# Second mixture: POOL no longer waits for its gather, and PE waits for the gathered rows itself

## The reference, cut to what matters

```
def _moe2_ref(x, w_skip, w_gate, w1, w2):          # x: 1536 x 512, 8 experts
    do_compute = (x @ w_skip) > 0
    out = x.copy()
    xc = x[do_compute]
    logits = xc @ w_gate
    e_idx = np.argmax(logits, axis=1)
    ... gate_w = softmax(logits)[e_idx]
    for e in range(8):
        mask = e_idx == e
        h = np.maximum(xc[mask] @ w1[e], 0.0)      # w1[e]: 512 x 1024
        y[mask] = gate_w[mask, None] * (h @ w2[e]) # w2[e]: 1024 x 512
    out[do_compute] = xc + y
```

## Time and profile before

| what | value |
|---|---|
| median of 3 runs | 729.18 us (725.63 to 731.9) |
| the profiled execution, its own time | 726.76 us |
| its span in the profile | 724.9 us |
| busy in the span | PE 90%, DVE 52%, ACT 40%, POOL 28% |
| second mixture | from 517.8 us to the end of the span |

### The profile page before, as it was taken

One profiled execution on the slowest core, in us unless ns is written; L12 is line 12 of the kernel. 1 busy time (PEld: TensorE's weight loads), 2 busy tenths in 40 slices (PEclk: granted clock), 3 DMA queues, 4 the chain that ended last, 5 costly groups with the idle time before them and its releaser, 6 DMA issues.

```text
span 724.9 us, 13743 instructions
## 1 busy us (share of the span) xinstructions
PE 653.6 (90%) x4192; PEld 577.0 (80%) x4192; DVE 375.6 (52%) x731; ACT 292.9 (40%) x503; POOL 205.8 (28%) x227
## 2 busy tenths in 40 slices
PE   5786884699999999999999999999699998999992
PEld 4675773389999999999999999976478876777771
DVE  2684697736364546345463645402574576636621
ACT  2362673024343444343343534405065474644620
POOL 0537580130241506051332415030022232221321
PEclk9898997599999999999999999999799999999997
DMA  9999996026272735537192827357355678557221
GB/s 192 204 223 237 267 291 230 20 80 206 75 215 68 185 132 126 201 80 247 50 258 68 219 73 187 129 97 217 96 198 179 178 255 268 152 146 261 44 43 16
DMA packets 94867, 116.16 MB, mean 160 GB/s; under 512 B 55940, under 2 KB 56068, under 8 KB 94800
## 3 DMA queue, kind: packets, MB, share of 16 engines
q1 hardware_dynamic: 77264, 90.83, 41.5%
q0 software_dynamic: 10464, 23.81, 15.7%
q10 hardware_dynamic: 7072, 0.71, 0.8%
HBM read 100.01 MB, written 20.18 MB: 166 GB/s over the span
## 4 chain that ended last, share of the span: by engine, by line
PE 57%; DMA 20%; SPq 8%; issue 7%; DVE 4%; POOLq 1%; POOL 1%; ACT 1%; DVEq 0%; ACTq 0%
PE bank L797 20%; PE bank L791 20%; DMA out<-y_sb,ix_put 10%; DMA xg<-x_moe,ix_take 8%; SPq L502 6%; PE bank L648 3%; PE bank L780 2%; PE bank L769 2%; SPq L517 2%; PE bank L720 2%; PE bank L698 1%; PE bank L681 1%; PE bank L710 1%; PE bank L898 1%; PE bank L670 1%
## 5 line engine op out<-in xcount | busy, mean ns | idle before, releaser
L1462 DVE TENSOR_TENSOR w_lo<-stage,w_hi x120 | 141.5, 1221 | 19.3 <-ACT w_hi L1022 17.4
L1022 ACT CAST w_hi<-stage x120 | 119.6, 1047 | 9.5 <-PE bank L898 9.4
L797 PE MATMUL bank<-unit_hi,w_hi 128*128 128x416 f32 x256 | 92.6, 362 | 0.0
L791 PE MATMUL bank<-tok_hi,w_hi 128*128 128x416 f32 x256 | 90.4, 353 | 0.0
L797 PE MATMUL bank<-unit_lo,w_hi 128*128 128x416 f32 x256 | 90.1, 352 | 0.0
L797 PE MATMUL bank<-unit_hi,w_lo 128*128 128x416 f32 x256 | 89.8, 351 | 0.0
L791 PE MATMUL bank<-tok_hi,w_lo 128*128 128x416 f32 x256 | 89.8, 351 | 0.0
L1696 DVE SCALAR_TENSOR_TENSOR unit_lo<-bank,unit_hi 128x416 fp32r<-128x416 f32 x64 | 37.9, 592 | 96.6 <-ACT unit_hi L1108 80.7
L1108 ACT ACTIVATE unit_hi<-bank 128x416 fp32r<-128x416 f32 x64 | 33.1, 518 | 128.6 <-PE bank L791 116.3
L1310 POOL DMA_INDIRECT x_moe<-rows_out,ix_put x32 | 58.8, 1837 | 53.3 <-DVE rows_out L1685 46.0
L791 PE MATMUL bank<-tok_lo,w_hi 128*128 128x416 f32 x256 | 58.5, 349 | 0.0
(11 more groups left out here) (163 smaller groups left out, 1114.6 us busy)
## 6 DMA issues: line engine op xcount, KB each, us to landing
stage<-in_moe_w SPq DMA_DIRECT2D x128, 512.0 KB, 6.2
v_win<-in_v SPq DMA_DIRECT2D x24, 192.0 KB, 6.6
x_moe<-rows_out SPq DMA_DIRECT2D x12, 260.0 KB, 4.0
x_att<-x_sb POOLq DMA_DIRECT2D x12, 256.0 KB, 5.2
x_sb<-x_moe SPq DMA_DIRECT2D x12, 256.0 KB, 2.8
out<-x_moe SPq DMA_DIRECT2D x4, 768.0 KB, 8.9
late_raw<-in_v SPq DMA_DIRECT2D x6, 384.0 KB, 7.6
stage<-in_k SPq DMA_DIRECT2D x6, 256.0 KB, 6.7
```

The costliest lines, as they stand in the source:

```text
L791: last = eng.matmul(ps_unit[f % 2][:, 0:W], w, x, start=(i == 0), stop=(i == len(mine) - 1))
L797: last = eng.matmul(ps_out[chunk][:, 0:W], w[:, WC // 2 + f, chunk * P:(chunk + 1) * P], h[:, f % UNITS, :], start=(f == 0 and i == 0), st ...
L1022: eng.copy(piece(w_hi[n % SETS], j), stage[:, j, :]).then_inc(s_hi, 1)
L1462: eng.tensor_tensor(piece(w_lo[n % SETS], j), stage[:, j, :], piece(w_hi[n % SETS], j).bitcast(F32), ALU.subtract)\
```

## The change

`take` no longer waits for its DMA. PE waits on the DMA's own semaphore `take` (16 per gather) in `turn_x`; the semaphore `taken` is gone. The copy of the token numbers into `ix_take` moves from before `take` into it, behind the waits for `xtp` and `gate`, because POOL's wait for the gather no longer guards `ix_take`. One wait for the last gather stands at the end of POOL's work.

```
@@ PE
                 def turn_x(ahead, n):
-                    eng.wait_ge(S["taken"], n + (ahead + 1))
+                    eng.wait_ge(S["take"], (n + (ahead + 1)) * 16)
                     if ahead:
                         eng.wait_ge(S["xte"], n + ahead)
@@ POOL
-                def take(n):
-                    eng.wait_ge(S["ixt"], n + 1)
+                def take(n, e, blocks):
                     eng.wait_ge(S["xtp"], n + 1)
                     eng.wait_ge(S["gate"], n + 1)
+                    eng.sem_inc(S["start"], 1)
+                    eng.tensor_copy(ix_take[:, 0:1], take_ix[:, e, blocks]).then_inc(S["ixt"], 1)
+                    eng.wait_ge(S["ixt"], n + 1)
                     eng.sem_inc(S["start"], 1)
                     eng.indirect_dma_start(xg[:], None, source, ...).then_inc(S["take"], 16)
-                    eng.wait_ge(S["take"], (n + 1) * 16)
-                    eng.sem_inc(S["taken"], 1)
@@ POOL's loop
-                        eng.tensor_copy(ix_take[:, 0:1], take_ix[:, e, bass.ds(dv, 1)]).then_inc(S["ixt"], 1)
-                        take(sv)
+                        take(sv, e, bass.ds(dv, 1))
                         with eng.If(eng.snap(slot, min_val=0, max_val=2 * NT + E) >= 2):
                             put()
@@ behind POOL's loop
-                eng.tensor_copy(ix_take[:, 0:1], take_ix[:, 0, 0:1]).then_inc(S["ixt"], 1)
-                take(eng.snap(slot, min_val=0, max_val=2 * NT + E))
+                last = eng.snap(slot, min_val=0, max_val=2 * NT + E)
+                take(last, 0, slice(0, 1))
                 for back in (2, 1):
                     with eng.If(eng.snap(slot, min_val=0, max_val=2 * NT + E) >= back):
                         put()
+                eng.wait_ge(S["take"], (last + 1) * 16)
```

More of the change, by code:

```diff
@@ L373, in build @@
             "take": "the slot's rows are gathered",
-            "taken": "Pool: it has seen them gathered",
             "xtp": "PE: they are transposed (one more than slots)",
```

## The result

The changed kernel takes **716.47 us** in the median of 4 runs (716.35 to 718.87), the kernel before 728.43 (725.63 to 731.9). The ratio is estimated at 0.9857, with a 95% interval of 0.9818 to 0.9896; the quotient of the two medians, 0.9836, lies inside it. The profiled execution took 716.35 us, its span is 714.5, so 10.4 us less than the 724.9 of before.

What follows compares the result with a forecast made beforehand. POOL's serial turn, 12.6 us against PE's 12.48, was taken as the bound. 9.49 + 2.5 = 12.0 us off 726.76 gives 714.8, or 717.2 if the runs' 2.4 us excess stays; middle 716.0, range 712.5 to 719.

Steps and rivals of the forecast that it cites:

- Part one: In the loop, POOL's wait for the gather goes, its turn falls from 12.6 to 9.2 us: -9.49 us.
- rival one: Partial gain: scatters land later behind a gather in flight, median 7.8 us as in the first mixture; 717 to 722, chance 0.14.
- the reserve: Spare time in POOL's turn of 9.2 us against PE's slot of 12.48: 3.3 us per slot.
- The pair of slots with splitting: Third expert's two successive splitting slots: ht_lo ready some 0.7 us before PE wants it; cost zero, bound 1.5 us.
- Part two: Copy of the token numbers behind POOL's waits: 0.2 to 1.1 us added before the gather, covered, value 0.
- A stop for the three pieces of 3.49 us: POOL held throughout DVE's splitting: scatter lands at 575.2, 1.3 us left rather than 2.4; sum still 12.0 us.
- Part three: PE waits on take itself at the transpose: value 0, bounds 0 and 0.5 us.
- Part four: At the end, the last y_sb starts right behind PE, its scatter no longer behind the unused gather: -2.5 us.
- Slower by serialised transfers: Rival two: each scatter queues behind its gather, landing above 8.3 us, POOL binds again; up to 770 us, chance 0.04.
- No effect: Rival three: POOL stands still at the scatter's issue until the gather is through; 727 to 729 us, chance 0.06.

Runs made afterwards that it cites:

- the last pair of runs: Kernel before and changed kernel, each with 28 fills of dead tiles on POOL between gather and scatter: 768.70 us and 724.59 us.
- the repeated run: The changed kernel once more, nothing altered, against the kernel before: 716.27 us, ratio 0.9849.
- the larger group: First group of follow-up runs: kernel before, median 727.27 us in 23 runs; the changed kernel once more, 716.27 us.

## Why the prediction was right

**The bound.** It was POOL's serial turn. The first and the last pair of runs show it from both sides: with the wait kept the gain is zero, and 3.2 us more per turn on POOL cost 39.9 us in the kernel before and about 8 in the changed one. One figure of this part was too low: POOL's instructions are 0.18 + 1.07 + 1.60 = 2.85 us a turn, not 2.5.

**Part one, 9.49 us in the loop.** It gave 8.2. The term I mis-sized was the scatter's landing. I took its median of before, 5.0 us, and got 6.0. That this comes with the missing wait is shown: with the wait kept the median is 5.0. What lengthens the landings is not settled. The gather in flight is not enough for it. Near the end of the stage a scatter 1.6 us behind its gather landed in 4.8 us, no later than the one of before that was issued at 708.25, behind a landed gather, in 4.8 too. The long landings, of 6.8 to 8.9 us, all lie where the 16 DMA engines were 76% to 98% busy, mostly with weights; the longest of before, 8.46 us, lay there too, at 96%. But others, at 79% to 87%, took 5.9 to 6.2 us. And the same scatter differs between two executions of the changed kernel. The timelines of POOL have it at 553.39 in the first, where it landed in 7.4 us, and at 550.74 in the repeated run, where it landed in 5.3:

```profile
553.39 2.46 POOL L1372 DMA_INDIRECT out<-y_sb,ix_put  x1 [0.31 <-issue]
```

```profile
550.74 1.60 POOL L1372 DMA_INDIRECT out<-y_sb,ix_put  x1 [0.31 <-issue]
```

Here the issue on POOL itself took 0.9 us more. So rival one's landings came, though not shown by its mechanism, and the reserve absorbed them in all slots but one. The slot of 13.71 us is the 1.2 us that was left, at the transpose. POOL's turn is still the scatter's landing plus 4.2 us, as I had it, but by luck: the scatter starts 0.31 us behind the gather's issue and not up to 1.34, and behind a late landing the next gather starts 2.2 to 2.8 us later and not 1.79. The pair of slots with splitting held: no wait of PE for `ht_lo` is left, so DVE's late work had been POOL's doing.

**Part two, the copy behind the waits, zero.** It now starts when `gate_next` is done, in three slots 1.2 to 1.5 us after the scatter before it has landed, and is covered; no run takes it alone. The gather's issue grew from 1.08 to 1.38 us in the rows above, and to at most 1.88, where it ran beside DVE's splitting. By the Trainium skill (SBUF — State Buffer, "Who interferes with whom") a DVE instruction with two inputs in SBUF contends with a GpSimd instruction that reads SBUF, and the trace agrees in kind. A stop for the three pieces of 3.49 us, which I had weighed as its full price, is not what the trace shows.

**Part three, PE's own wait, zero.** Shown by the kernel in which POOL tells PE ahead of the scatter's landing, with the full gain. What I had not said is that the place of the word matters as much as the place of the wait: behind the scatter's landing it costs the whole gain.

**Part four, 2.5 us at the end.** It gave 2.2 between the last rounding and the end of the span; the last `y_sb` moved by 2.7 and the time behind the last scatter grew by 0.5 us. The size was right and the reason was not. I put it down to the scatter queued behind the unused gather, but that wait put back costs nothing measurable. POOL had come late to its last turns: the unused gather was issued 5.3 us ahead of the last rounding before, and 10.5 us ahead of it now. The lateness was what stood at the end.

**Sum and level.** 8.2 + 2.2 = 10.4 us in the profiled executions, for 12.0 forecast. That the median came out 0.5 us from the forecast is partly luck. The gain was 1.6 us smaller. Against it I had added 1.2 us, half of what the profiled run of before stood below its median, and the changed kernel's median lies only 0.1 us above its profiled run. The medians themselves differ by 12.0 us in the first four runs of each, and by 11.0 in the larger group. In the profiled runs of all kernels here the first rounding lies between 523.1 and 528.7 us, before the change can act. Between the two profiled runs of the changed kernel it differs by 2.4 us, and their times by 2.2. So there the difference was made earlier; for the other runs this is not shown.

**The rivals.** Partial gain: I priced it at 719 from the profiled execution (726.76 - 7.3 = 719.5); on the forecast's own footing it would have been 720.7. Slower by serialised transfers: the scatter's landings had a median of 6.0 us, below the 8.3 from which POOL would bind, and only one, of 8.9, was above it. The Trainium skill's section "Two DMAs through the same engine are not ordered" (DMA: Bandwidth & Descriptors) has descriptors start in order but pipelined. The landings agree: the gather at 690.12 landed in 3.5 us, 1.9 us behind the start of the scatter at 691.73, and the scatter still landed in the 4.8 us of one alone. No effect: excluded.

## What to carry to other kernels

An engine that waits for each of its own transfers has a turn that is the sum of its latencies. Add that turn up and compare it with the pace of the bound engine: here 12.6 against 12.48 us hid behind a POOL that was 28% busy over the whole execution. When such a wait is moved, check both who is freed and who hears: the consumer's word must not end up behind another transfer. A load put on the suspected engine tells a bound from a bystander, if the trace shows that the load really lengthened its turn.

## What the runs showed of the hardware that I had not expected

Four POOL fills of together 0.9 us, placed between a wait and an indirect DMA, delayed that DMA by 0.1 us: from landing to start were 1.45 us with them and 1.34 without. Of 28 fills, 4.2 us long, 3.2 us were added. And a scatter issued earlier need not land earlier: with twelve fills ahead of it, it started 3.1 us behind its gather rather than 1.4, and landed at 560.2 us rather than 560.8, at the same point of the stage to within 0.2 us.
